# RWKV-style attention with two dense layers, one core: attention levels computed on narrow column tiles of TensorE, both batches of a level together

## What is computed

```python
for t in range(S):
    cur = einsum('bhd,bhe->bhde', u * k[t], v[t])
    y[t] = einsum('bhd,bhde->bhe', r[t], state + cur)
    state = w[t] * state + einsum('bhd,bhe->bhde', k[t], v[t])
x = y                                   # 3072 x 384
x = (sigmoid(x @ w_gate) * (x @ w_val)) @ w_out      # d_ff 1536
h = x @ w_in; out = elu(h) @ w_out2                  # d_ff 2048
```

## Time and profile before

| | |
|---|---|
| median of 3 runs | 1154.9 us (1153.87 to 1155.38) |
| profiled execution, its own time | 1155.4 us |
| its span in the trace | 1153.7 us |
| mean granted TensorE clock | 0.987 |
| PE / PEld busy | 1100.6 / 976.4 us |
| DVE / ACT / POOL busy | 637.0 / 491.9 / 260.9 us |
| level products, L575 | 1152 records, 158.3 us busy |

### The profile page before, as it was taken

How to read it: one execution, slowest core, us unless ns; L and a number is a source line. 1 busy time by engine, 2 the same in 40 slices (tenths; PEclk the granted TensorE clock), 3 DMA queues, 4 the chain that set the end, 5 groups by cost and what they waited for, 6 DMA issues and landing times.

```text
span 1153.7 us, 17839 instructions
## 1 busy us (share of the span) xinstructions
PE 1100.6 (95%) x6972; PEld 976.4 (85%) x6972; DVE 637.0 (55%) x938; ACT 491.9 (43%) x943; POOL 260.9 (23%) x258
## 2 busy tenths in 40 slices
PE   5587899999999999999999999999999999999998
PEld 4586899888888888888888888889999998999998
DVE  6676679494839484947495733353434333343433
ACT  2434444433343334334433433364545444454543
POOL 8222256161506250625062500000000000000000
PEclk9799899999999999999999999999999999999999
DMA  6627142431414041403140041220101001010000
GB/s 123 104 68 143 44 66 35 67 51 26 62 42 59 18 63 42 60 18 63 42 62 15 1 138 58 66 83 1 55 1 55 2 1 55 1 55 1 28 1 28
DMA packets 154324, 54.84 MB, mean 48 GB/s; under 512 B 115968, under 2 KB 151936, under 8 KB 154240
## 3 DMA queue, kind: packets, MB, share of 16 engines
q1 hardware_dynamic: 154240, 53.70, 22.7%
HBM read 39.52 MB, written 9.44 MB: 42 GB/s over the span
## 4 chain that ended last, share of the span: by engine, by line
PE 84%; DVE 7%; ACT 3%; issue 3%; SPq 2%; DMA 1%; DVEq 0%; ACTq 0%
PE ps L631 23%; PE ps L664 17%; PE ps L656 17%; PE ps L640 10%; PE ps L575 9%; PE ps L565 3%; DVE RKW L839 2%; PE ps L591 2%; PE ps L597 2%; ACT RKW L685 1%; DVE A L871 1%; SPq L359 1%; DVE work L934 1%; DVE WS L944 1%; ACT hh L685 1%
## 5 line engine op out<-in xcount | busy, mean ns | idle before, releaser
L631 PE MATMUL ps<-xh,WS 128*128 128x512 f32 (+1 forms) x1008 | 257.1, 374 | 19.3 <-DVE xl L919 10.9
L685 ACT ACTIVATE hh<-work 128x512 fp32r<-128x512 f32 (+1 forms) x180 | 108.7, 604 | 283.0 <-DVE work L934 200.2
L631 PEld LDWEIGHTS ps<-xh,WS 128*128 128x128 f32 x1008 | 172.4, 193 | 45.6 <-DVE WS L944 9.4
L664 PE MATMUL ps<-WS,hh 128*128 128x384 f32 x768 | 195.5, 335 | 0.6 <-DVE hl L923 0.6
L923 DVE TENSOR_TENSOR hl<-work,hh 128x512 fp32r<-128x512 f32 (+1 forms) x180 | 131.3, 729 | 89.3 <-ACT hh L685 89.2
L575 PEld LDWEIGHTS ps<-RKW 128*128 128x128 f32 x1152 | 151.0, 196 | 26.0 <-DVE RKW L839 18.8
L640 PE MATMUL ps<-hh,WS 128*128 128x512 f32 (+1 forms) x504 | 164.8, 375 | 6.6 <-DVE hl L923 6.4
L575 PE MATMUL ps<-RKW 128*128 128x128 f32 x1152 | 158.3, 282 | 12.3 <-DVE RKW L839 10.7
L499 POOL TENSOR_TENSOR RKW<-RKW,WL 128x256 f32<-128x256 f32 x144 | 128.5, 893 | 173.8 <-PE ps L575 173.1
L656 PE MATMUL ps<-xh,WS 128*128 128x512 f32 x576 | 161.3, 392 | 0.0
L961 DVE SCALAR_TENSOR_TENSOR work<-work,ps 128x512 f32<-128x512 f32 x96 | 66.0, 687 | 164.4 <-ACT work L787 164.4
(11 more groups left out here) (67 smaller groups left out, 1190.7 us busy)
## 6 DMA issues: line engine op xcount, KB each, us to landing
nat<-in_w_dram SPq DMA_DIRECT2D x24, 192.0 KB, 3.6
nat<-in_k_dram SPq DMA_DIRECT2D x24, 192.0 KB, 4.9
nat<-in_r_dram SPq DMA_DIRECT2D x24, 192.0 KB, 5.3
V<-in_v_dram SPq DMA_DIRECT2D x24, 192.0 KB, 4.8
x_scratch<-work SPq DMA_DIRECT2D x12, 384.0 KB, 3.0
nat<-x_scratch SPq DMA_DIRECT2D x6, 768.0 KB, 6.2
out_dram<-A SPq DMA_DIRECT2D x5, 768.0 KB, 4.3
xs<-yT SPq DMA_DIRECT2D x72, 48.0 KB, 2.0
```

Of the source, the lines that this page charges most:

```text
L631: last = mm(ps[:, VAL if val else GATE, t], gate_w(a, val, j, c), xp[b][:, c, t], start=(i == 0 and c == 0), stop=(i == 2 and c == KC - 1))
L664: last = mm(ps[:, ACC2 + b, 0:HD], hp[ap][:, j % 2, b * P:(b + 1) * P], down2_w(wp, j), start=(j == 0 and i == 0), stop=(j == F2 - 1 and i ...
L685: return nc.scalar.activation(o, i, ACT.Copy)
```

## The change

Levels 1 to 4 are computed in four tiles of 32 keys: a block of at most 32 steps lies inside one tile, so a tile needs the queries of its own 32 steps only, 16 in second halves for each head, 32 columns. Level 5 has two tiles of 64 keys with 64 columns. Level 6 takes the 64 keys of the first half and streams the 64 queries of the second, one head into each half of the output partitions. The output is 32 or 64 columns a pair, so both batches of a level fit into one bank; S of both batches also shares one. Level products of batch 1 follow those of batch 0 at once, with the dense thirds of both behind them. The masks are put in by four operations on 32 partitions with both batches in each, after batch 1; ACT's copies take both batches.

```diff
+    COLS = {li: HP // 2 if 2 ** li <= HP // 4 else HP for li in range(1, NL - 1)}
+    def shares(name):
+        return name[0] == "L" or name == "S"
+    FILLS = [use for use in USES if not (shares(use[2]) and use[3] > 0)]
+    FILL_OF = {use: x for x, use in enumerate(FILLS)}
...
-        return ATTN + PLACE_OF[use] % NBK
+        _, q, name, b = use
+        return ATTN + FILL_OF["a", q, name, 0 if shares(name) else b] % NBK
...
     EVEN = {**{(name, b): 1 for name in STAGES for b in range(U)},
+            **{(f"L{li}", b): 2 * b for li in range(1, NL) for b in range(U)},
             ("KT", 1): 3, ("Y", 0): 0, ("Y", 1): 0, ("S", 0): 0, ("S", 1): 2}
     SHORT = {...
+             **{(f"L{li}", b): 2 * x * b for li, x in ((1, 5), (2, 5), (3, 5), (4, 4), (5, 2.5), (6, 2.5)) for b in range(U)},
...
-                    for p, g in enumerate(pairs):
-                        Rb = R[:, :, g].rearrange("q e (i two l) -> q e i two l", two=2, l=L)
-                        last = mm(bank[:, p * P:(p + 1) * P].rearrange("p (e i l) -> p e i l", e=2, l=L),
-                                  K[:, g, :], Rb[:, :, :, 1, :], start=True, stop=True)
+                    if li < NL - 1:
+                        C = COLS[li]
+                        for g in pairs:
+                            for c in range(P // C):
+                                own = slice(c * C, (c + 1) * C)
+                                Rb = R[:, :, g, own].rearrange("q e (i two l) -> q e i two l", two=2, l=L)
+                                last = mm(bank[own, g * C:(g + 1) * C].rearrange("p (e i l) -> p e i l", e=2, l=L),
+                                          K[:, g, own], Rb[:, :, :, 1, :], start=True, stop=True)
+                    else:
+                        for g in pairs:
+                            for e in range(2):
+                                last = mm(bank[e * L:(e + 1) * L, g * L:(g + 1) * L], K[:, g, 0:L], R[:, e, g, L:P],
+                                          start=True, stop=True)
...
+                    if b == 1:
+                        act.wait_ge(d_mask, masked(q, NM - 1))
+                        if li < NL - 1:
+                            C = COLS[li]
+                            src = bank[:, 0:G * C].rearrange("p (x i l) -> p x i l", x=2 * G, l=L)
+                            for s0 in range(0, P, 2 * L):
+                                last = copy(A[s0:s0 + L, :, :, s0 + L:s0 + 2 * L].rearrange("p g e t -> p (g e) t"),
+                                            src[s0:s0 + L, :, s0 % C // (2 * L), :])
+                        else:
+                            for e in range(2):
+                                last = copy(A[0:L, :, e, L:P], bank[e * L:(e + 1) * L, :].rearrange("p (g t) -> p g t", g=G))
...
                     next_level_r(q, li, b)
-                    if li < NM:
-                        nc.vector.copy_predicated(
...
+                    if b == 1 and li < NM:
+                        C = COLS[li]
+                        for c in range(TILES[li]):
+                            own, half = slice(c * C, (c + 1) * C), slice(c * C // 2, (c + 1) * C // 2)
+                            nc.vector.copy_predicated(
+                                blocks(A[own, :, :, own].rearrange("p g e t -> p (g e) t"), L)[:, :, :, 1, :],
+                                masks[own, li, half].bitcast(I32).rearrange("p (i l) -> p i l", l=L).unsqueeze(1)
+                                .to_broadcast([C, 2 * G, C // (2 * L), L]),
+                                bank[own, 0:G * C].rearrange("p (x i l) -> p x i l", x=2 * G, l=L)).then_inc(d_mask, 1)
```

More of the change, by code:

```diff
@@ L278, in level, with masked @@
             return 2 * n * q + 2 * li + b + 1
+        TILES = {li: P // COLS[li] for li in range(1, NM)}
+        def masked(q, li):
+            return q * sum(TILES.values()) + sum(TILES[x] for x in TILES if x <= li)
         def w1_raw(x):
@@ L512, in attention @@
                 elif name == "KT" and b == 1:
-                    wait(pool, d_s, 4 * q)
+                    wait(pool, d_s, 2 * q)
                     for e in range(2):
@@ L604, in attention @@
                         for e in range(2):
-                            last = mm(bank[e * HP:e * HP + D, p * D:(p + 1) * D], KM[:, g, e * HP:e * HP + D],
+                            last = mm(bank[e * HP:e * HP + D, g * D:(g + 1) * D], KM[:, g, e * HP:e * HP + D],
                                       V[:, hf, g, e, :], start=True, stop=True)
@@ L706, in attention @@
                     L = 2 ** li
-                    act.wait_ge(d_mask, level(q, NM - 2, b, NM - 1))
+                    bank = ps[:, bank_of("a", q, name, b), :]
                     act.wait_ge(s_att, count("a", q, name, b))
-                    src = ps[:, bank_of("a", q, name, b), :].rearrange("p (x i l) -> p x i l", x=2 * PR, l=L)
-                    for i in range(P // (2 * L)):
-                        s0 = 2 * L * i
-                        last = copy(A[s0:s0 + L, b * PR:(b + 1) * PR, :, s0 + L:s0 + 2 * L].rearrange("p g e t -> p (g e) t"),
-                                    src[s0:s0 + L, :, i, :])
-                    last.then_inc(a_score, 1)
+                    if b == 1:
[9 more added lines that the diff above has]
+                                last = copy(A[0:L, :, e, L:P], bank[e * L:(e + 1) * L, :].rearrange("p (g t) -> p g t", g=G))
+                        last.then_inc(a_score, 1)
                     if li == NL - 1:
@@ L866, in attention @@
                         dve.wait_ge(p_zero, 4)
-                    if 1 < li < NM:
-                        dve.wait_ge(d_mask, level(q, li - 2, b, NM - 1))
                     next_level_r(q, li, b)
-                    if li < NM:
-                        nc.vector.copy_predicated(
-                            blocks(A[:, pairs].rearrange("p g e t -> p (g e) t"), L)[:, :, :, 1, :],
-                            masks[:, li, :].bitcast(I32).rearrange("p (i l) -> p i l", l=L).unsqueeze(1)
-                            .to_broadcast([P, 2 * PR, P // (2 * L), L]),
-                            bank.rearrange("p (x i l) -> p x i l", x=2 * PR, l=L)).then_inc(d_mask, 1)
+                    if b == 1 and li < NM:
+                        C = COLS[li]
+                        if li > 1:
+                            dve.wait_ge(d_mask, masked(q, li - 1))
+                        for c in range(TILES[li]):
[5 more added lines that the diff above has]
+                                bank[own, 0:G * C].rearrange("p (x i l) -> p x i l", x=2 * G, l=L)).then_inc(d_mask, 1)
                     if name == "L4" and b == 0:
@@ L901, in attention @@
                         near[:, 2 * b * PR:2 * (b + 1) * PR].unsqueeze(2).to_broadcast([P, 2 * PR, i, 2])).then_inc(d_diag, 1)
-                elif name == "S":
+                elif name == "S" and b == 1:
                     dve.wait_ge(p_sw, 2 * (q + 1))
                     dve.wait_ge(s_att, count("a", q, name, b))
-                    new = bank[:, 0:PR * D].rearrange("p (g d) -> p g d", g=PR)
+                    new = bank[:, 0:G * D].rearrange("p (g d) -> p g d", g=G)
                     for e in range(2):
                         rows = slice(e * HP, e * HP + D)
-                        tt(ST[rows, hf, pairs, e, :], SW[rows, pairs, :], new[rows], ALU.add).then_inc(d_s, 1)
+                        tt(ST[rows, hf, :, e, :], SW[rows], new[rows], ALU.add).then_inc(d_s, 1)
                 for li in DECAYS.get((name, b), []):
```

22 lines of the change are left out of this document (10 added, 12 removed).

## The result

The changed kernel takes 1175.3 us (median of 4 runs, 1169.95 to 1178.9) beside 1155.1 for the kernel before: a ratio of 1.016, 95% interval 1.013 to 1.019. It is slower by 20 us where the prediction had 26 less; the range is missed too. The profiled execution took 1175.65, its span is 1173.9.

What follows compares the result with a forecast made beforehand. TensorE was taken as the limit in quarters 2 to 11: (1.7 + 1.0 + 0.3) x 10 = 30 us, less 3 for quarters 2 and 3, plus 3 for quarters 0 and 1, 4 kept back: -26, 1129 us; range 1120 to 1160.

Steps and rivals of the forecast that it cites:

- What is moved: Between levels, batches together: waits for R go, counted 0.3 us a quarter; masks add 0.6 on VectorE, hidden.
- the frame: Quarters 2 to 11: TensorE is the limit, so what it is spared shortens the run almost one for one.
- rival 3: Levels 1 to 4: 32-column tiles do not overlap, 32 ns a record, +8 us, 1163 us; chance 0.15.
- rival 1: Levels 1 to 4: start limit of 22.5 ns a record, so no gain there, 1139 us; chance 0.22.
- the 16 ns a record: Levels 1 to 4: extrapolated price of 32-column records; 1.38 us a level against 1.81, 1.7 us gained a quarter.
- the way in and out: Around each of six levels a quarter: entering and leaving narrow tiles costs 0.36 us, bounds nothing and twice as much.
- 64 columns: Levels 5 and 6: 29 ns a record, 1.29 us a level, a gain of 0.52 each, 1.0 a quarter.
- Masks: On VectorE: operations of 256 elements cost 0.4 us each, 0.7 at level 1.
- The tail: After the last S: as long as before.
- quarters 0 and 1: Start of the run: about -2 us in quarter 0 and -1 in quarter 1, together -3 us.
- Rival 2: VectorE's R, R and four masks unbroken: h or hl reaches PE late, 1.1 us a quarter, 1143 us; chance 0.12.
- The clock: Granted clock, low only in two of 40 slices before 145 us and full after: no term moved on it.

Runs made afterwards that it cites:

- e7: Changed kernel with the two batches of level 1 as far apart as before, levels 2 to 6 together: 1163.7 us, ratio 1.009.
- e1: Changed kernel with its tiles, shared banks and masks, but batches of a level two thirds apart as before: 1151.2 us, ratio 0.996.
- e9: Kernel before, full-width level products, with more dense work between levels 1 to 4 of full sets and less elsewhere: 1151.1 us, ratio 0.996.
- e8: Changed kernel with batches apart as before, more dense work between levels 1 to 4 of full sets and less elsewhere: 1130.2 us, ratio 0.978.
- e2: Kernel before, full-width level products, with the batches of a level together as in the change: 1163.3 us, ratio 1.005.

## Why the prediction was wrong

**The step that failed** is in "What is moved": "the long POOL term falls beside the masks and no longer beside an R product. I therefore expect the waits for R to go." I listed the order of each engine's steps and not their times. Level 1's masks were priced at 0.7 each; four of them with `hl` are 3.5 us, more than the four thirds (2.7 us) between levels, and that alone puts the next R pair beside GpSimd's next term. Measured: masks and `hl` 3.97 us, an R pair of 3.42 us, and waits for R of 41.9 us instead of none.

**The second step missed** is not in the text at all: that batch 1 of level 1 needs its own transposed r, and that the two thirds ahead of it covered ScalarE's copies. It is a wait of 2.17 us in quarter 7, and e7 puts such waits, with what they lead to, at 12 us.

**The third** is the frame. I read 118.84 of 120 us as "therefore shortens the run almost one for one", and had beside it, in the earlier trace rows, a VectorE at 13.90 of 13.90 us in levels 1 to 3. Both were true: the two paths were nearly equal there, and an engine spared beside an equal one gains only what separates them. e1 and e9 say it from both sides: tiles alone 4 us, places alone 4 us, both 25 (e8). Two quarters can be summed: 114.3 before, less 1.2 idle, less 2 x 4.7 spared, is 103.7 us of work; TensorE is idle for 8.1 us of each 120, 7.8 in 116; and at a mean granted clock of 0.97 a further 3.5 are lost: 115.0 of the 116.0 measured (an estimate from these rows; what is missing is at least in part waits too short to show as idle time: level 5 of quarter 7 costs 1.63 us by the starts instead of 1.29).

**Right or only mis-sized.** Tiles overlap (rival 3 fell; its sign came true for another reason). There is no start limit at S's 22.5 ns (rival 1 fell: 9 ns). 32 columns cost 0.90 us a level, priced 1.38: the term that was mis-sized is the 16 ns a record, a price for two tiles at once. It was 9, close to the 8 that the prediction named as the bound for four; the way in and out was 0.30, charged 0.36. 64 columns cost 1.29 as priced. Masks measured 0.44 at the median and 0.76 at level 1, priced 0.4 and 0.7. The tail did not change. For quarters 0 and 1 I had -3 us and it was +9.4. Level 4 of quarter 1, forecast 2.1 us earlier, came at 99.69 us where batch 1's stood at 94.36, behind the waits for `hl`, and so the weight piece came later too and not sooner.

**Rival 2** (VectorE's block too long) named the mechanism, VectorE's long block: it came true with two waits for `hl` in quarter 1, and later with waits for R and not, as the text had it, for h or `hl`. It was sized by the longest stall of the kernel before, one of 1.1 us a quarter. There are 3.9 us a quarter of them, at a TensorE that had 2 us a quarter less to do than priced, and 1.7 more by the clock; it should have ended on the slower side. **The clock** was in no term: "I move no term on it". Before, it stood at 1.00 from 300 us on, beside 1.2 us idle in 120. In the changed kernel, idle for 8.1 us, it fell once a quarter for 3.4 us. In e1, idle for 5.5 us with one wait of 2.33, it stayed at 1.00.

What stays open: why quarter 1 with pairs and tiles loses 8.3 us and e2, pairs at full width, only 1.4. TensorE's waits behind its first dense record there add up to 19.0 us, in e2 to 13.3 and before to 11.8, and the clock between 60 and 100 us is 0.76, 0.90 and 0.99; no run here separates the two. No run moves `hl` ahead of the masks either, so how much the mere order of VectorE's queue costs is not shown.

## What to carry to other kernels

When an edit makes the bounding engine faster, look up how busy the engine that feeds it is in the same stretch, not in the whole run; if it is near full there, the gain is what separates them, until the work around the stage is spread so that its longer path is covered (here the same tiles gave 4 us at the old places and 21 at wider ones). Before an order of steps is called better, lay out the starts of each engine with durations for one stage, above all which instruction stands beside the neighbour's long one, and for each second half of a pair ask what it alone still waits for. Waits that leave TensorE idle can cost more than their length: behind some of them, not all, the clock fell here.

## What the runs showed of the hardware

- *Four tiles of 32 columns in turn take 9 ns a record* (0.90 us for a level of 64 records, 0.60 for a group of 32), with their weight loads beside them. The Trainium skill (TensorE: Matmul & The Clock Gate, "Wait — 56ns, not 53.3ns?") was cited in rival 1 for a floor of about 25 ns from start to start; the measurement decides: where four tiles of the array take turns, even the two records of one matmul take less than that, 19 ns.
- *GpSimd holds up a VectorE product of two SBUF inputs however small it is*: three products of 32, 16 and 8 elements went from 0.60 to 2.95 us, in which two terms of about 2 us ran.
- *A way in and out of narrow tiles costs 0.3 us at 32 columns* (2 x 0.60 - 0.90), near the 0.36 around Y and S.
- *After some short waits the dense records of the next 3.4 us start 0.42 us apart instead of 0.23*: behind two of 2.17 and 1.75 us and behind two of 1.03 and 0.77, but not behind the first of these alone, and not behind one of 2.33 in e1.
